# Three expert blocks ahead of the last chunk's gate, front and experts in one program

## What is computed

```python
x = attention(q, k, v)          # 8 heads of 64; 4 sinks and a causal window of 128
h = x @ w_in                    # 512 -> 2048
x = (h - tanh(h)) @ w_out       # 2048 -> 512
logits = x @ w_gate + modality_bias[modality_id]
e = argmax(logits)              # one of 8 experts for each token
gate = softmax(logits)[e]
out[token] = gate * (relu(x[token] @ w1[e]) @ w2[e])   # 512 -> 1024 -> 512
```

## Time and profile before

| | us |
|---|---|
| median of 3 runs (1161.42 to 1161.92) | 1161.58 |
| the profiled execution | 1163.88 |
| its span in the trace | 1162.3 |
| PE busy | 1023.1 (88%) |
| DVE busy | 729.9 (63%) |
| ACT busy | 619.6 (53%) |
| POOL busy | 398.9 (34%) |

### The profile page before, as it was taken

One profiled execution on the slowest core, in us unless ns is written; L12 is line 12 of the kernel. 1 busy time (PEld: TensorE's weight loads), 2 busy tenths in 40 slices (PEclk: granted clock), 3 DMA queues, 4 the chain that ended last, 5 costly groups with the idle time before them and its releaser, 6 DMA issues. The chain is left out here.

```text
span 1162.3 us, 24476 instructions
## 1 busy us (share of the span) xinstructions
PE 1023.1 (88%) x7840; PEld 669.8 (58%) x7840; DVE 729.9 (63%) x2388; ACT 619.6 (53%) x1421; POOL 398.9 (34%) x463
## 2 busy tenths in 40 slices
PE   1767888999999999999999999998178999779997
PEld 0534545665665665665665666563166777557774
DVE  6787868678877777977867866465533333433332
ACT  2776866675676765766766766454023322332231
POOL 3796776223253422345322320101112232213222
PEclk9978989999999999999999999999579999889999
DMA  9831112321321341212212300210142111011111
GB/s 287 253 98 36 34 33 48 96 69 34 78 47 33 61 120 34 60 37 61 61 33 65 60 2 1 101 73 1 36 173 43 45 53 46 27 28 50 48 47 44
DMA packets 24537, 74.32 MB, mean 64 GB/s; under 512 B 10176, under 2 KB 10304, under 8 KB 22912
## 3 DMA queue, kind: packets, MB, share of 16 engines
q1 hardware_dynamic: 15056, 59.79, 19.5%
q0 software_dynamic: 5792, 13.43, 3.7%
q10 hardware_dynamic: 3600, 0.03, 0.2%
HBM read 60.17 MB, written 13.33 MB: 63 GB/s over the span
## 5 line engine op out<-in xcount | busy, mean ns | idle before, releaser
L759 PE MATMUL acc<-w_out_all,g_hi 128*128 128x512 f16 x768 | 228.4, 379 | 0.0
L703 PE MATMUL h_ps<-xt_hi,w_in_all 128*128 128x384 f16 x1024 | 211.6, 330 | 16.3 <-DVE g_raw L724 16.3
L759 PE MATMUL acc<-w_out_all,g_lo 128*128 128x512 f16 x384 | 145.6, 379 | 3.2 <-DVE g_lo L744 1.7
L591 ACT ACTIVATE pt_hi<-pt_ps 128x256 f16<-128x256 f32 (+2 forms) x224 | 83.6, 380 | 110.5 <-PE pt_ps L608 106.4
L703 PEld LDWEIGHTS h_ps<-xt_hi,w_in_all 128*128 128x128 f16 x1024 | 97.9, 99 | 77.2 <-DVE g_raw L724 14.7
L97 POOL TENSOR_TENSOR tick<-tick 1x1 f32<-1x1 f32 x87 | 16.1, 185 | 325.3 <-DVE payload L879 113.1
L744 DVE SCALAR_TENSOR_TENSOR g_lo<-g_raw,batch_scale,g_hi 128x384 f16<-128x384 f32 x128 | 95.2, 743 | 33.2 <-ACT g_hi L734 30.7
L759 PEld LDWEIGHTS acc<-w_out_all,g_hi 128*128 128x128 f16 x768 | 75.0, 98 | 69.3 <-issue 0.2
L715 ACT ACTIVATE g_raw<-h_ps,batch_scale 128x384 f32<-128x384 f32 x128 | 74.3, 580 | 75.7 <-PE h_ps L703 74.4
L595 DVE TENSOR_TENSOR pt_lo<-pt_ps,pt_hi 128x256 f16<-128x256 f32 (+2 forms) x224 | 94.3, 423 | 29.8 <-ACT pt_hi L591 28.2
L429 POOL TENSOR_TENSOR q_stack<-qk_raw,q_stack 64x768 f16<-64x768 f32 x31 | 50.8, 1639 | 165.1 <-ACT q_stack L425 165.1
(11 more groups left out here) (261 smaller groups left out, 2234.1 us busy)
## 6 DMA issues: line engine op xcount, KB each, us to landing
qk_raw<-in_qk SPq DMA_DIRECT2D x64, 454.0 KB, 6.0
raw<-in_w SPq DMA_DIRECT2D x16, 512.0 KB, 8.4
v_raw<-in_v SPq DMA_DIRECT2D x4, 1536.0 KB, 9.8
x_tokens<-x SPq DMA_DIRECT2D x24, 256.0 KB, 5.6
w_in_all<-in_w_in SPq DMA_DIRECT2D x4, 1024.0 KB, 13.1
w_out_all<-in_w_out SPq DMA_DIRECT2D x4, 1024.0 KB, 12.0
slot_g<-slots POOLq DMA_DIRECT2D x27, 1.0 KB, 2.1
xg<-x_tokens,slot_g POOLq DMA_INDIRECT x27, 3.4
```

The source lines that it names most:

```text
L591: eng.activation(pt_hi[:, at, :], out, ACT.Copy).then_inc(q["pt_hi_done"], 1)
L703: mm = eng.matmul(h_ps, w16[0][:, f, x * DM + k * P:x * DM + (k + 1) * P], r[:, par, k, :], start=(i == 0), stop=(i == 3 * KD - 1))
L759: mm = eng.matmul(acc[t][:, :], l[f % 2][:, t * P:(t + 1) * P], w16[1][:, f, x * DM:(x + 1) * DM], start=(f == 0 and i == 0), stop=(f == N ...
```

## The change

The function `experts` becomes `expert_stage`, which is called inside `front` and returns its steps, so that there is one program and no boundary. Its PSUM banks are those of the front (transposes in `x_bank`, hidden in the two `pt_bank`, output in `h_bank` and `acc[0]`); its x, hidden and y tiles lie over the attention's buffers. Three blocks (`EARLY = 3`) of the first expert, from tokens that the first six chunks have routed, become blocks 0, 1 and 2:

- `first_expert` takes six more DVE steps: it counts the tokens that can be had (`taken`, at most 384) and the row where the rest begins. POOL loads their rows with one DMA and, when chunk 6 is stored, gathers the three blocks into `xe`. SP stores chunk 7 only behind these gathers. The zero fill of x2 at the start covers the last chunk's rows too.
- In the last window, slots 23 to 27 reduce and scale the three blocks, slots 28 to 31 transpose blocks 0 and 1. `prepare_expert` now stands ahead of `mlp_evacuate` in a slot.
- `gate_last` puts block 0's 96 hidden products on PE as 24 ahead of the chunk's transposes, 24 behind them, 48 behind the logits; relu halves stand between choice and ranking and behind it.
- `join` runs `early_iteration` 1 and 2 on PE, with the plan cut into three on DVE between relus, then `joining_iteration`: block 2's output alone, block 3's hidden products alone. POOL waits for all scatters and stores, then loads rows and gathers block 3. The loop starts at j = 4 and reads the table at j - 3. SP's late weight loads stand behind its store waits.
- The plan subtracts `taken` from the first expert's count and keeps its turn active. The semaphores of the weight pieces become one counter for each half.

The diff, cut to its core:

```diff
+EARLY = 3
...
+            if k == 23:
+                stage_e.early_top(E, eng, 0)
+                stage_e.early_top(E, eng, 1)
+            if k == 25:
+                stage_e.early_top(E, eng, 2)
+                stage_e.early_scales(E, eng)
+                stage_e.early_scale(E, eng, 0)
+            if k == 27:
+                stage_e.early_scale(E, eng, 1)
+                stage_e.early_scale(E, eng, 2)
+            if (k, E) in ((28, "pe"), (29, "act"), (29, "dve")):
+                if E == "pe":
+                    eng.wait_ge(q["xt_lo_done"], HP * NC)
+                stage_e.transpose_x(E, eng, 0, 0)
+            if (k, E) in ((30, "pe"), (31, "act"), (31, "dve")):
+                stage_e.transpose_x(E, eng, 1, 1)
 
         def gate_last(E, eng, g):
...
             if E == "pe":
+                early = stage_e.hidden_products(eng, 0, 0)
+                eng.wait_ge(q["pt_lo_done"], 7 * HP * NC)
...
+                some(24)
+                for t in range(TPC):
...
+                    for k in range(KD):
+                        mm = eng.transpose(acc[t][:, k * P:(k + 1) * P], x2[t][:, k * P:(k + 1) * P], ident[:])
+                    mm.then_inc(q["x2t_done"], 1)
+                some(24)
                 claim_scores(eng)
...
+                some(48)
...
+                stage_e.relu(E, eng, 0, 0)
...
             gate_choose(E, eng, g)
+            if E == "dve":
+                stage_e.relu(E, eng, 0, 0)
             gate_rank(E, eng, g)
+
+        def join(E, eng):
+
+            if E == "pe":
+                eng.wait_ge(q["logits"], TPC * NC)
+                stage_e.early_iteration(E, eng, 1, 1)
+                eng.wait_ge(q["x2t_copied"], TPC * NC)
+                stage_e.early_iteration(E, eng, 2, 0)
...
+            if E == "dve":
+                stage_e.relu(E, eng, 0, 1)
+                shared.plan(E, eng, counts)
+                stage_e.relu(E, eng, 1, 0)
+                stage_e.transpose_x(E, eng, 2, 0)
+                shared.plan_blocks(eng)
+                stage_e.relu(E, eng, 1, 1)
+                stage_e.relu(E, eng, 2, 0)
+                shared.plan_late(eng)
+            if E == "pool":
+                eng.wait_ge(q["scattered"], 16 * TPC * NC)
+                eng.wait_ge(q["x2_st"], 16 * TPC * NC)
+                stage_e.load_slots(E, eng, EARLY)
+                stage_e.gather(E, eng, EARLY)
+                stage_e.early_iteration(E, eng, 1, 1)
+                stage_e.early_iteration(E, eng, 2, 0)
+            stage_e.joining_iteration(E, eng)
+            stage_e.blocks(E, eng)
...
+                eng.wait_ge(stage_e.q["gathered_e"], 16 * EARLY)
+                mlp_store(E, eng, NC - 1)
...
+                eng.wait_ge(q["scattered"], 16 * TPC * (NC - 2))
+                stage_e.early_rows(E, eng)
+                eng.wait_ge(q["x2_st"], 16 * TPC * (NC - 1))
+                stage_e.early_gathers(E, eng)
...
+        step(tt(count[:, 0:1], count[:, 0:1], self.taken[:], ALU.subtract))
...
+    def early_scales(E, eng):
+
+        if E == "dve":
...
+            step(ts(xe_exp[:], xe_top[:].bitcast(I32), 255 * EXP1, None, ALU.bitwise_and))
+            step(ts(xe_exp[:], xe_exp[:], float(2 * EXP1), float(253 * EXP1), ALU.max, ALU.min))
+            ts(xe_scale[:].bitcast(I32), xe_exp[:], -1.0, float(255 * EXP1), ALU.mult, ALU.add).then_inc(q["xe_set"], 1)
+            step(ts(xe_undo[:].bitcast(I32), xe_exp[:], float(-EXP1), None, ALU.add))
+            step(ts(xe_undo[:], xe_undo[:], shared.undo[:, 0:1], None, ALU.mult))
+            for b in range(EARLY):
+                eng.tensor_tensor(ye_scale[:, b:b + 1], slot_e[:, b, 1:2].bitcast(F32), xe_undo[:, b:b + 1], ALU.mult)\
+                   .then_inc(q["y_set"], 1)
...
+    def joining_iteration(E, eng):
+
+        j, p = EARLY, EARLY % 2
+        if E == "pe":
+            for _ in output_products(eng, j - 1, 1 - p, j - 2):
+                pass
+            transpose_x(E, eng, j, p)
+            for _ in hidden_products(eng, j, p):
+                pass
+            transpose_x(E, eng, j + 1, 1 - p)
...
+        if E == "pool":
+            load_slots(E, eng, j + 1)
+            gather(E, eng, j + 1)
+            output(E, eng, j - 1, 1 - p)
+            load_slots(E, eng, j + 2)
+            gather(E, eng, j + 2)
```

More of the change, by code:

```diff
@@ new lines, in gate_last, with some @@
+                eng.wait_ge(q["pt_lo_done"], 7 * HP * NC)
+                def some(count):
+                    for _ in range(count):
+                        next(early)
+                some(24)
+                for t in range(TPC):
+                    if t == 1:
+                        eng.wait_ge(q["evac_dve"], g + 1)
+                    else:
+                        eng.wait_ge(q["evac_act"], 2 * g + (1 if t == 0 else 2))
+                    for k in range(KD):
+                        mm = eng.transpose(acc[t][:, k * P:(k + 1) * P], x2[t][:, k * P:(k + 1) * P], ident[:])
+                    mm.then_inc(q["x2t_done"], 1)
@@ L933, in gate_last @@
+                score_readers[:] = [(q["logits"], n + TPC)]
+                some(48)
+            if E == "act":
+                for t in range(TPC):
                     eng.wait_ge(q["x2t_done"], n + t + 1)
@@ L939, in gate_last @@
                     if t == 2:
[L940 to L953, removed]
+                        eng.wait_ge(q["h_done"], NF * NC)
@@ L1219, in program @@
             window(E, eng, NC - 1, i)
+            if E == "act":
+                eng.nop().then_inc(stage_e.q["y_out"], 1)
             gate_last(E, eng, NC - 1)
-            shared.plan(E, eng, counts)
-            if E == "pool":
-                eng.wait_ge(q["scattered"], 16 * TPC * NC)
+            join(E, eng)
         with nc.Block("front") as block:
@@ L1795, in experts @@
-        with nc.Block("experts") as block:
-            @block.sync
-            def _(eng):
-                program("sp", eng)
-            @block.scalar
-            def _(eng):
-                program("act", eng)
-            @block.vector
-            def _(eng):
-                program("dve", eng)
-            @block.gpsimd
-            def _(eng):
-                program("pool", eng)
-            @block.tensor
-            def _(eng):
-                program("pe", eng)
+        if E in ("act", "dve"):
+            relu(E, eng, j - 1, 1)
+            relu(E, eng, j, 0)
+            if j + 1 < EARLY:
+                transpose_x(E, eng, j + 1, 1 - p)
+            output(E, eng, j - 1, 1 - p)
@@ new lines, in last_output @@
+    def last_output(E, eng, last, regular):
+        if E == "pe":
+            eng.wait_ge(q["y_set"], last)
+            for _ in output_products(eng, last, 0, last):
+                pass
+        if E == "act":
+            relu(E, eng, last, 1)
+            load_slots_again(E, eng, last)
+            output(E, eng, last, 0)
+        if E == "dve":
+            relu(E, eng, last, 1)
+            output_part(E, eng, last, last % 2, turn_of(eng, last))
+            output_scale(E, eng, last, regular + 1)
+        if E == "pool":
+            output(E, eng, last, 0)
+            eng.wait_ge(q["gathered"], 16 * (regular + 3))
+            eng.wait_ge(q["scattered"], 16 * (last + 1))
@@ new lines, in late_loads, with blocks @@
+    def late_loads(eng):
+        eng.wait_ge(shared.planned_late, 1)
+        turns = read(eng, 3, NB, NE, lo=1)
+        with eng.Fori(1, NE) as s:
+            with eng.If(s < turns):
+                load_turn(eng, s)
+    def blocks(E, eng):
+        eng.wait_ge(shared.planned, 1)
+        regular = read(eng, 1, MB - 1 + EARLY, NB - 1, lo=1)
+        last = regular + EARLY
+        eng.wait_ge(shared.planned_late, 1)
+        with eng.Fori(0, (NB + 5) // 8) as g:
+            with eng.If(8 * g + EARLY + 1 <= last):
+                with eng.Fori(4 * g + (EARLY + 1) // 2, 4 * g + (EARLY + 1) // 2 + 4) as i:
+                    j = 2 * i
+                    with eng.If(j <= last):
+                        iteration(E, eng, j, 0, j - 2)
+                        with eng.If(j + 1 <= last):
+                            iteration(E, eng, j + 1, 1, j - 1)
+        last_output(E, eng, last, regular)
@@ L1828, in build @@
             front(nc, dram, shared, attention)
-        experts(nc, dram, shared)
 def kernel(**inputs):
```

613 lines of the change are left out of this document (327 added, 286 removed).

## The result

| | before | after |
|---|---|---|
| median, us | 1161.75 (4 runs, 1161.42 to 1162.04) | 1142.72 (4 runs, 1138.62 to 1143.85) |
| profiled execution, us | 1163.88 | 1141.86 |
| span, us | 1162.3 | 1140.2 |

The ratio is 0.983 with a 95% interval of 0.9804 to 0.9855: faster, by 19.0 us between the medians and by 22.0 us between the profiled executions. The forecast was 1136.0 in a range of 1128.5 to 1143.0; the time lies in the range, 6.7 us above the point. The gain is real and smaller than forecast.

The account below looks back on a forecast made before the run. PE was taken as the bound, with a hole between front and experts. Moving three iterations gives -33.0, the later loop start (864.6 - 857.24) leaves -25.6 us: 1136.0 against the median, range 1128.5 to 1143.

Parts of the forecast that it names:

- The hole: Between front and experts PE waits for scaled x, idle from 821 to 844; three iterations, 33.0 us, move in.
- rival 3: Early iterations: DVE's order makes PE wait, half of the 23.5 us wait stays; some -14, 1148 us; chance 0.06.
- The window: Last chunk: early steps at slots k=23, 25, 30 add 1.4, 0.8, 1.1 us before its last output products, together 3.3.
- Gate and early iterations: After the last chunk's products: logits at 819.6, PE goes on at 825.7, two iterations end at 847.3.
- The join: Before the loop: block 4's rows take 2.28 us, its gather lands at 861.0, the loop starts at 864.6, not 857.24.
- rival 2: Block 4's rows and gather queue behind the weight pieces; gather near 864.5, start 868.2: -22.0, 1139.6 us; chance 0.12.
- Rival 1: Block 4's gather isn't held up by the weight pieces, lands at 857.9, clock stays full: -31.4, 1130.2 us; chance 0.17.
- From landing to the first product: Block 4's gather landing to the loop's first output product: taken as 3.65 us, as before.
- The clock: PE at 0.50 after its pause before the loop: a cost of 2.2 us, kept unchanged on both sides.
- Behind the join: From the loop's first iteration on: same look-ahead, weight turn and tail, with three iterations, 33.0 us, fewer.
- rival 4: Loop: extra register work above 1.5 us in each of 21 iterations loses the gain; at 2 us, 1173; chance 0.03.
- The fill: Startup zero fill of x2 grows fourfold, in a store awaited by nothing near; no cost in the sum.

Follow-up runs that it names:

- The rearranged kernel: Changed kernel with block 4's tokens in block 0's buffer, rows and gather before weight pieces, early steps spread, loop bounds read early: 1133.42 us, ratio 0.9773.
- the experiment with the rows first: Changed kernel with block 4's row load alone moved ahead of block 1's scatter, and so of the weight pieces: 1137.78 us, ratio 0.9819.

## Why the prediction was right, and where it was off

- **The hole, right.** What was said to bound the kernel did, and rival 3 is out: PE is busy 28.36 of 29 us from 821 to 850 and waits for no relu longer than 0.64.
- **The window, right in the sum, by luck in its parts.** The last output products start at 813.43 against 813.5: 3.25 later in place of 3.3. The forecast had 1.4 at k=23, 0.8 at k=25 and 1.1 at k=30; measured were 1.12, 0.63 and 0.72. The difference was made up by two costs that were not in the sum: 0.28 at the window's start, where the six more steps of DVE had been taken as 0, and 0.43 for block 0's transposes on PE. The rearranged kernel shows that the waits could be had back.
- **Gate and early iterations, right.** Logits 819.37 (819.6), the first early iteration 825.60 (825.7), block 2's output alone from 847.1 (847.3), the last step of the ranking at 827.1 (828).
- **The join, the step that failed.** The 2.28 for rows and "the gather lands between 857.9 and 862.0" were the mis-sized terms. The row load took 5.9, so the gather went out at 856.09 in place of 854.5; it took 8.39 in place of 6.5, and landed at 864.48, 3.5 later than forecast and outside both bounds; the sign named for being right, a gather of 5 to 8 us, was missed with it. I had priced the pieces for the gather and not for the row load ahead of it, on the ground that "rows go out only 2 us after the pieces" (it was 1.0); the experiment with the rows first gains 3.4 us by that alone. The mechanism is rival 2's, given 0.12, with 864.5 for the landing and 868.2 for the start, measured 864.48 and 868.70. That its landing fits to the hundredth is luck: it had the rows near 858, which left the gather 6.5, and they came at 855.7, with a gather of 8.39. Its reason, that the rows are as many packets as the tokens, is not so: alone in the trace of before, a row load moved 32 packets (836.0 to 838.4) and a gather 80 (838.4 to 842.0). A row to price it by was in hand: the 7.54 of the earlier trace rows is a transfer of POOL issued 3.1 us behind the pieces.
- **Rival 1's rule.** The Trainium skill's sentence (DMA: Bandwidth & Descriptors, "Queues, rings and completion order") that each DMA engine alternates between queue rows packet by packet was read as letting POOL's transfers pass with little delay. The runs don't bear that reading out: beside the pieces the rows took 5.9 in place of 2.16, the gather 8.39 and 9.04 in place of 4.89. In which order the engines took the packets no run here shows.
- **From landing to the first product**, 4.22 against 3.65. Of it 0.82 is the loop's entry, 0.27 in the earlier trace rows; the 0.55 between them were not in the sum.
- **The clock, about right.** After the pause the first four pairs of the iteration take 3.48 us, from 868.70 to 872.18, in place of 4 x 0.44; 1.7 us are lost where I kept 2.2 (granted clock 0.50 from 866 to 870). The 2.2 was read from seven pairs in the earlier trace rows; there are six from 857.24 to 863.03, so that before the clock cost some 2.5, an estimate from these rows.
- **Behind the join, right.** 33.6 against 33.0, with 11.0 an iteration and no wait for y_scale in the steady loop: rival 4 is out.
- **The fill, taken as 0.** "Awaited by nothing near" holds, and yet the medians put it at 1.1 to 3.3 us. It may be part of what the medians lack beyond the join; that is argued from medians, and the two profiled executions reach chunk 6 at the same 743.78.

So of 6.7 us, 3.6 are the join (4.1 later, 0.6 given back behind it), and 3.1 come from carrying the profiled execution's offset to the median; how much of them is the fill isn't shown.

## What to carry to other kernels

When idle time is filled by moving work forward, the wait turns up at the next transfer that could not move: price every transfer of that chain (index rows as well as data) against whatever bulk load the change now releases at the same moment. Put the small transfers ahead of the bulk load and give them their own buffer, rather than hold the bulk load back, which moved the collision to the next block here; the traces put the difference at 1.8 us at the end of the span, the medians don't show it. And a step placed on a busy engine costs what stands in queue behind it: the same steps in other slots gave about 2 us back (2.9 at the end of the span, less the 1.0 of the loop's entry).

## What the runs showed of the hardware

- A small transfer of POOL beside eight 512 KB loads of SP was slowed: 128 table rows, 2.0 to 2.3 us without the loads, took 5.9; a 256 KB gather, 3.40 to 4.89 without the loads, took 7.30 to 9.04.
- Entering the loop cost PE 0.82 to 1.38 us in which it waited for nothing that the profile shows, and 0.42 once the loop's bounds had been read earlier.
- In the front, PE's work from one row to the next took 5.70 us with granted clock 0.50 from 56 to 58 us and 4.20 at 1.00. Chunk 6 came at 743.8 with the one and with the other, so this shows no cost for the whole.
